# Retention stage of a routed two-layer kernel: row-half scores, decays moved to values and output, diagonal state, routing in groups of blocks

## The reference

```python
# 1 retention, per batch b (2), head h (8), 768 steps, head_dim 64
gamma = 1.0 - 2.0 ** (-5.0 - arange(8))
state = gamma * state + outer(k[t], v[t])
y[t]  = (1 / sqrt(64)) * q[t] @ state
# 2 one expert of eight per token (D 512, F 1024), in token order
fresh = argmax(logits[s])
e     = fresh if s == 0 or local_gate[s] < 0.5 else previous e
out[s] = softmax(logits[s])[e] * relu(x[s] @ w1[e]) @ w2[e]
# 3 four attention experts, top two mixed
```

## Time and profile before

| | us |
|---|---|
| median of three runs | 480.01 |
| lowest and highest run | 478.17, 480.32 |
| span of the profiled execution | 478.0 |
| busy PE, DVE, ACT, POOL | 430.0, 298.3, 211.8, 115.2 |
| the longest chain: PE, DVE, issue, DMA | 74%, 11%, 7%, 4% |

### The profile page before, as it was taken

The page is one execution under the profiler, slowest core; times in us unless marked ns, Lnnn a source line. Parts: engine busy times, 40 slices in busy tenths (PEclk is TensorE's granted clock), DMA queues, the critical chain, the costliest instruction groups (busy, mean ns, idle before and its releaser), DMA issues.

```text
span 478.0 us, 9620 instructions
## 1 busy us (share of the span) xinstructions
PE 430.0 (90%) x3060; PEld 382.2 (80%) x3061; DVE 298.3 (62%) x677; ACT 211.8 (44%) x413; POOL 115.2 (24%) x126
## 2 busy tenths in 40 slices
PE   3899999934999999999999999579979899979887
PEld 2888888824989898989898999379957689967675
DVE  2599999974656565656565654254788841687860
ACT  1123322253346464646464646134555643455653
POOL 1546556320110000000000000170049600014340
PEclk9999999965999999999999999969989999998999
DMA  7987566227777767677776791162400011220003
GB/s 245 300 272 213 180 217 240 106 101 280 236 257 257 263 219 263 224 258 234 256 249 206 240 346 50 49 194 78 121 0 2 2 62 73 66 66 0 0 0 132
DMA packets 32723, 78.37 MB, mean 164 GB/s; under 512 B 4032, under 2 KB 4160, under 8 KB 32704
## 3 DMA queue, kind: packets, MB, share of 16 engines
q1 hardware_dynamic: 25888, 58.21, 37.6%
q0 software_dynamic: 4512, 15.73, 9.7%
q10 hardware_dynamic: 2304, 4.20, 2.3%
HBM read 57.67 MB, written 17.30 MB: 157 GB/s over the span
## 4 chain that ended last, share of the span: by engine, by line
PE 74%; DVE 11%; issue 7%; DMA 4%; ACT 2%; POOL 1%; SPq 1%; DVEq 0%; ACTq 0%; POOLq 0%
PE bank L1188 7%; PE bank L1189 7%; PE bank L1190 7%; PE bank L1205 6%; PE bank L1203 6%; PE bank L1204 6%; PE bank L1303 4%; PE bank L1288 4%; PE bank L1273 2%; PE bank L1082 2%; PE bank L1168 2%; PE bank L1249 2%; PE bank L1247 2%; PE bank L1248 2%; PE bank L1274 2%
## 5 line engine op out<-in xcount | busy, mean ns | idle before, releaser
L1188 PE MATMUL bank<-xh,w1h 128*128 128x256 f32 x256 | 73.5, 287 | 0.9 <-DVE xl L901 0.9
L1189 PE MATMUL bank<-xl,w1h 128*128 128x256 f32 x256 | 73.3, 286 | 0.0
L1190 PE MATMUL bank<-xh,w1l 128*128 128x256 f32 x256 | 73.2, 286 | 0.0
L895 DVE TENSOR_TENSOR w2l<-raw,w2h 128x1024 fp32r<-128x1024 f32 x32 | 37.2, 1222 | 43.0 <-ACT w2h L581 43.0
L518 POOL TENSOR_SCALAR att<-att,stat,mixw 128x128 f32<-128x128 f32 (+5 forms) x48 | 34.1, 718 | 95.0 <-DVE stat L1037 95.0
L581 ACT ACTIVATE w2h<-raw 128x1024 fp32r<-128x1024 f32 x32 | 31.5, 1049 | 47.8 <-PE bank L1205 45.6
L1188 PEld LDWEIGHTS bank<-xh,w1h 128*128 128x128 f32 x256 | 50.0, 195 | 1.3 <-DVE xl L901 1.0
L1203 PE MATMUL bank<-w2h,hh 128*128 128x512 f32 x128 | 50.6, 395 | 0.0
L1189 PEld LDWEIGHTS bank<-xl,w1h 128*128 128x128 f32 x256 | 50.1, 196 | 0.3
L1190 PEld LDWEIGHTS bank<-xh,w1l 128*128 128x128 f32 x256 | 50.0, 195 | 0.0
L1205 PE MATMUL bank<-w2h,hl 128*128 128x512 f32 x128 | 49.9, 390 | 0.0
(11 more groups left out here) (155 smaller groups left out, 975.5 us busy)
## 6 DMA issues: line engine op xcount, KB each, us to landing
raw<-in_w SPq DMA_DIRECT2D x64, 512.0 KB, 6.5
xr<-tokens_by_expert POOLq DMA_DIRECT2D x8, 512.0 KB, 4.1
outputs_by_expert<-ysb ACTq DMA_DIRECT2D x16, 256.0 KB, 5.7
tokens_by_expert<-zero POOLq DMA_DIRECT2D x7, 512.0 KB, 6.2
q_in<-in_qT SPq DMA_DIRECT2D x12, 256.0 KB, 2.8
kz_in<-in_kT SPq DMA_DIRECT2D x24, 128.0 KB, 4.1
k_in<-in_kR SPq DMA_DIRECT2D x12, 256.0 KB, 3.9
v_in<-in_vR SPq DMA_DIRECT2D x12, 256.0 KB, 4.1
```

The costliest lines, as they stand in the source:

```text
L895: dve.tensor_tensor(part(low), raw[:, q, :], part(high).bitcast(F32), ALU.subtract).then_inc(w_lo, 1)
L1188: pe.matmul(to, w1h[:, dc, at], xh[:, dc, :], start=(dc == 0), stop=False)
L1189: pe.matmul(to, w1h[:, dc, at], xl[:, dc, :], start=False, stop=False)
L1190: last = pe.matmul(to, w1l[:, dc, at], xh[:, dc, :], start=False, stop=(dc == DC - 1))
```

## The change

- Scores: the keys are loaded without zeros (`kt_in`), and each head's product has 64 rows, in partitions 0 to 63 or 64 to 127. The heads of a pair go to banks 0 and 1. DVE multiplies all eight heads by one causal mask, in one instruction of 1024 columns.
- Decays: gamma^-s is put on the values by ACT (`v_dec`, eight activations of 64 columns), gamma^t and the scale on the output by DVE, in place of ACT's copy to `xT`. POOL's two multiplications are gone.
- State: 64 x 64 for each head, 256 columns instead of 512. Keys times values and state times queries are eight products of 64 columns or 64 x 64 each instead of four full ones. No state is formed for the last block of a batch, and none read for the first.
- Routing in groups of blocks (0-2, 3-5, 6-8, 9-10, 11). A group's fresh choice is made one block after its last, its scans two blocks after, its places three blocks after. The scans run over up to 384 tokens. The probabilities are computed for all blocks at once, after the first tile is split.
- `xT` and `state` are rings of two, `xrow` is a ring of four.
- POOL writes zeros to the first 256 rows of the token list at the start, and the first tile is loaded when the scatters have landed; the first expert's pad, at row 256 at the earliest, follows. Five zero writes of 512 KB to the outputs, two of SP and three of POOL before, are all on SP's queue behind the first weights.
- The decay constants are 0.35 MB instead of 1.3 MB.

```diff
-        pe.matmul(bank[:, h // 4, ...], kz_in[:, s, par, hp * P:(hp + 1) * P], q_in[:, s, ...])
+        own = half_rows(par)
+        last = pe.matmul(bank[:, par, at], kt_in[own, s, at], q_in[own, s, at], start=True, stop=True)
...
+            def state_out(i):            # 8 products, 64 rows x 64 columns, 128 wide
+                pe.wait_ge(state_ready, states_before(i))
+                        pe.matmul(bank[own, 3, hp * P:(hp + 1) * P], state[own, i % 2, hp, :],
+                                  q_in[own, i % RING, hp * P:(hp + 1) * P], ...)
...
+            for i in range(NB):          # TensorE
+                block_scores(i)
+                if i >= 1:
+                    rows_and_gates(i - 1)          # waits xT_ready i, xrow_ready i-1
+                if i - 2 in closing:
+                    turn_fresh(closing[i - 2])
+                if i - 3 in closing:
+                    turn_places(closing[i - 3])
+                chunk_out(i)                       # state_out(i), then probs x v_dec
+                if i % C < C - 1:
+                    block_kv(i)
+            last_g = len(GROUPS) - 1
+            rows_and_gates(NB - 1)
+            turn_fresh(last_g - 1)
+            turn_places(last_g - 1)
+            turn_fresh(last_g)
+            turn_places(last_g)
...
+            for i in range(NB):          # VectorE
+                mask_scores(i)
+                if i >= 1:
+                    sum_gates(i - 1)
+                block_x(i)
+                if i % C < C - 1:
+                    block_state(i)
+                if i - 1 in closing:
+                    fresh_choice(closing[i - 1])
+                if i - 2 in closing:
+                    count_places(closing[i - 2])
+                if i - 3 in closing:
+                    read_places(closing[i - 3])
...
+            def token_rows(j):           # ScalarE
+                act.wait_ge(gates_ready, j + 1)
+                if j >= XRING:
+                    act.wait_ge(scattered[j % XRING], 16 * (j // XRING))
+                act.activation(xrow[:, j % XRING, :]...).then_inc(xrow_ready, 1)
+            for i in range(1, NB + 1):
+                token_rows(i - 1)
+                if i - 2 in closing:
+                    kept(closing[i - 2])
+                if i + 1 < NB:
+                    decay_values(i + 1)
...
+            for g, (a, z) in enumerate(GROUPS):    # GpSimd
+                pool.wait_ge(pos_ready, g + 1)
+                for j in range(a, z):
+                    pool.wait_ge(xrow_ready, j + 1)
+                    pool.indirect_dma_start(xs, ... posi[:, j:j + 1] ..., xrow[:, j % XRING, :], None)
...
+            for s in range(XRING):                 # SyncE
+                sp.wait_ge(scattered[s], 16 * NB // XRING)
+            sp.dma_start(xr[:, :, :], rows(xs, 0, TILE)...).then_inc(first_tile_in, 16)
             sp.wait_ge(pads_ready, 1)
             sp.dma_start(rows(xs, r, TILE)..., zero[:, :]).then_inc(first_padded, 16)
-            sp.wait_ge(first_padded, 16)
-            sp.dma_start(xr[:, :, :], rows(xs, 0, TILE)...).then_inc(first_tile_in, 16)
```

More of the change, by code:

```diff
@@ L150, in build_kernel @@
[L150 to L160, removed]
+        state = sb("state", [P, 2, HP, HD])
@@ L382, in load_w1 @@
+            for i in range(2, NB):
+                load_turned(i)
+                load_plain(i)
             def load_w1(e, q):
@@ L529, in _, with decay_values @@
         def _(act):
+            def decay_values(i):
+                s, to = i % RING, i % 2
+                act.wait_ge(chunk_in[s], 32 * (i // RING) + 32)
+                if i >= 2:
+                    act.wait_ge(y_done, i - 1)
+                    act.wait_ge(kv_done, states_before(i - 1))
+                for h in range(H):
+                    at = slice(h * HD, (h + 1) * HD)
+                    last = act.activation(v_dec[:, to, at], v_in[:, s, at], ACT.Copy, scale=lead[:, L_KD + h:L_KD + h + 1])
+                last.then_inc(v_ready, 1)
@@ L564, in _ @@
-            with act.Fori(1, NB // RING) as k:
-                for s in range(RING):
-                    i = RING * k + s
-                    token_rows(i - 1, (s - 1) % RING, k - 1 if s == 0 else k)
-                    exps(i - 2, (s - 2) % RING)
-                    route(i - 2, (s - 2) % RING)
-                    retention(i, s)
-            token_rows(NB - 1, RING - 1, NB // RING - 1)
-            exps(NB - 2, RING - 2)
-            route(NB - 2, RING - 2)
-            exps(NB - 1, RING - 1)
@@ new lines, in chunk_out @@
+            def chunk_out(i):
+                pe.wait_ge(xT_ready, i)
+                if i % C:
+                    state_out(i)
+                pe.wait_ge(probs_ready, i + 1)
+                pe.wait_ge(v_ready, i + 1)
+                for hp in range(HP):
+                    for par in range(2):
+                        h = 2 * hp + par
+                        last = pe.matmul(bank[half_rows(par), 3, hp * P:(hp + 1) * P],
+                                         v_dec[:, i % 2, h * HD:(h + 1) * HD], probs[:, par * HP + hp, :],
+                                         start=(i % C == 0 and hp == 0), stop=True, skip_group_check=True)
+                last.then_inc(y_done, 1)
@@ new lines, in block_kv @@
+            def block_kv(i):
+                s = i % RING
+                pe.wait_ge(chunk_in[s], 32 * (i // RING) + 32)
+                pe.wait_ge(state_ready, states_before(i))
+                for hp in range(HP):
+                    for par in range(2):
+                        at = slice((2 * hp + par) * HD, (2 * hp + par + 1) * HD)
+                        last = pe.matmul(bank[half_rows(par), 2, hp * HD:(hp + 1) * HD], k_in[:, s, at],
+                                         v_dec[:, i % 2, at], start=True, stop=True)
+                last.then_inc(kv_done, 1)
@@ L1175, in _ @@
             pe.wait_ge(delta_ready, 1)
-            pe.matmul(bank[:, 7, 0:E], ones[0:1, :], over[0:1, 0:E], start=True, stop=True).then_inc(ey_done, 1)
+            pe.matmul(bank[:, 7, 0:E], ones[0:1, 0:P], over[0:1, 0:E], start=True, stop=True).then_inc(ey_done, 1)
             with pe.Fori(0, E) as e:
```

556 lines of the change are left out of this document (252 added, 304 removed).

## The result

The changed kernel takes 486.38 us (median of 4 runs, 484.02 to 488.18), the kernel before 480.16 on the same chip. The ratio is 1.0131, its 95% interval 1.0090 to 1.0171: slower, by about 6 us. The profiled execution took 484.02 us with a span of 482.4, against the span of 478.0 before. Device times of its runs lie 1.5 to 1.6 us over their spans.

A forecast was written before the change was run, and what follows sets the result against it. Either PE or DVE was taken to set the pace from 41 to 84 us. Start -7.0, middle +6.2 and tail +6.0 gave +5.2, span 478.0 to 483.2, plus 2.0 to the median: 485.2 us, range 474 to 494.

The forecast's parts named there:

- The ring wait: Middle: PE's rows of blocks 5 and 8 wait until scatters free `xrow` slots; stalls of 3.4 and 3.5 us.
- The crowding at block 8: Middle, block 8: first weights and five zero writes in flight lengthen the stall by 1.0 us.
- Start: Up to the end of block 0's output: ends at 11.7 instead of 18.68 us, a gain of 7.0.
- Products: PE's products and turns from block 0's to block 11's output: 64.1 us, with scores at 1.5 a block.
- The middle: End of block 0's output to end of block 11's: 76.9 us before clock losses, 83.0 with them, a loss of 6.2.
- stalls for places: Middle: PE's turn_places waits for DVE's counting, 1.55 us three times, 4.7 in all.
- half clock: Middle: slowed clock costs 2.2 us behind each of two stalls and 1.7 from the start, 6.1 us.
- Tail: Block 11's output to the experts' first product: 26.8 us against 20.8, a loss of 6.0.
- Rival 1: Scores and stage clock: halves overlap whole, scores take 1.02 us and the clock holds; 475 us, chance 0.27.
- Rival 3: State products: a pair's heads don't overlap, 1.8 instead of 1.0 us ten times; 493 us, chance within a shared 0.10.
- Rival 4: Start: scores wait for something else and the 7.0 us gain shrinks; +3 us, chance within a shared 0.10.

The follow-up runs named there:

- the ring of six: The changed kernel with six slots for `xrow` instead of four: 461.85 us, ratio 0.9629 to the kernel before.
- the groups of two: The changed kernel with routing in six groups of two blocks, `xrow` still four slots: 470.54 us; with weights and zero writes also held back, 466.95 us.
- the weights held: The changed kernel with the first expert's weights and the zero writes issued only after the scatters of blocks 1 and 5 landed: 483.09 us.
- the run with both changed: The ring of six, with ACT no longer waiting for plain keys before scaling the first values and its table loaded earlier: 462.66 us.
- busy work in the stalls: The changed kernel with unused identity products on PE before rows_and_gates of blocks 5, 8 and 11: 483.83 us.
- after: The changed kernel itself, with the whole change against the kernel before: 486.38 us, ratio 1.0131.

## Why the prediction was right

The sign, the place and the size were right: 485.2 predicted, 486.38 measured. That it came so close is in part luck. The start gained 2.6 us less than predicted, the middle lost 2.1 less and the tail 1.4 less. Inside the middle the products came out 10.0 us shorter and the ring stalls 6.8 us longer than predicted. The mechanism, saved products that come back as waits for a slot, is what the runs show.

- **The ring wait decides**: shown, by the ring of six (20.7 us of waits for ACT's copy to none, 24.5 us of time) and by the groups of two. Its size at block 5 was 5.4 against the 3.4 predicted: from block 5's output DVE's steps ahead of the scatter took 1.7 (1.0 predicted), the scatter 4.0 (3.2) and the copy 0.75 (0.66), and PE's scores ahead of the wait were shorter (1.1, not 1.5), which lengthens a stall that ends at a fixed moment. At block 8 it was 9.5 against 3.5 and the 1.0 for crowding.
- **The crowding at block 8** was the worst-sized term: 1.0 predicted, 4.6 less in the stall with the weights held (3.3 in the time). I charged it as a small share of 16 us of traffic; the scatter started just behind 2 MB of weights and took 8.4 us from start to release.
- **Start**: 4.4 gained, not 7.0. The scores took 2.08 us, 2.85 predicted, but I took the scaled values as ready. I had not read what ACT's wait asks for, nor looked for the table load behind it; the run with both changed had the output at 11.97. (The prediction's steps add up to 11.6 and not 11.7.)
- **Products.** Scores 1.09: row halves overlap nearly whole (the bound was 1.02), 4.5 us in eleven blocks. Keys times values 0.56, not 1.0: 4.4 us. Values times scores 0.92, 1.4 us. The turns took 0.75 each, 0.6 less in all; rows and state were 0.9 over. In all 54.1, or 10.0 us less than my 64.1.
- **The middle** then closes: 54.1 of products, 4.35 of stalls for places (1.37, 1.49, 1.49; predicted 4.7), 14.9 of ring stalls (8.1 predicted), and 7.6 left for half clock and small gaps (6.1 predicted): 80.9. Rows at half the clock make 5.8 of this: 0.7 behind block 0, 1.4 where the clock fell at 39.4, 1.6 behind each of the two ring stalls, and 0.5 at 94.1. So a stall cost 1.6 in slow rows and not 2.2, the start 0.7 and not 1.7, and two falls of the clock lay where I had none. Against the ring of six the middle is longer by 80.9 - 62.9 = 18.0, the two stalls and 3.1 beside their length. Of that, busy work in the stalls won back 2.5 at most: ACT's queue is late there too.
- **Tail** 25.4 against 26.8, along the steps predicted: rows 5.84 after block 11's output (5.95), two counts, the last scatter 15.7 after it (16.8). The 1.4 us less come from the first count and its turn, over at T + 12.0 and not at 13.1.
- **Rival 1** (halves overlap whole, the clock holds) was half right: they overlap, the clock didn't hold, and every product shortened ahead of a ring stall came back in the stall. The 3.4 us that it gives to the scores don't follow from its own numbers: 0.48 in eleven blocks is 5.3, and half of it 2.6.
- **Rival 3** is refuted. State times queries of a pair's two heads, in two opposite quarters of the array, both write bank 3. Sixteen records take 1.03 us, 64 ns each, as line 1105 did, and in the trace's single records the products of a pair start 7 ns apart, the next pair 110 ns later. The Trainium skill, TensorEngine Tiling (Array Packing), Gotcha 1: PSUM Pressure, says that different row tiles cannot access one bank at once; the measurement differs, for products of 64 x 64. Nor do loads of 128 columns into different row halves follow one another: sixteen scores' loads take 0.97 us, where the prediction's estimate from the Trainium skill, TensorE: Matmul & The Clock Gate, LDWEIGHTS, was 1.7.
- **Rival 4** came true in small, for a reason that I had not named: what ACT waits for, and its table, cost some 2.4 us of the start.

What stays open: why the clock falls where it does (at 55.7 and 76.2 in the run that had started 2.4 us earlier, at 84.5 in the ring of six); and how much of a scatter's landing, 2.7 to 8.5 us, is chance (block 0's took 4.0 and 5.5 us to its release in two kernels with the same program up to there).

## What to carry to other kernels

When work is grouped, a buffer is released later by the length of the group and by all that follows it: recount every ring against the new latest release, in blocks. Here four slots for groups of three made three stalls of 20.7 us together, about what the products of the middle save (PE is busy with them for some 75 us before and 54 after), and two more slots were worth 5%. Holding back a crowding transfer can move the crowding to the next small one, as with groups of two. Read each semaphore wait of a moved operation for what it asks beyond its operands, and look up which transfers are issued just ahead of a small one that something waits for.

## What the runs showed of the hardware

- Two products of 64 rows in different row halves overlap, weight loads of 128 columns too: sixteen records in 1.09 us (68 ns each), against 1.88 us with 128 rows. The two of a pair start 6 to 7 ns apart, the next pair 110 ns later, and with 128 rows each record starts 112 ns behind the one before. Keys times values, 64 columns wide on either side, takes 35 ns a record.
- POOL's multiplication slowed DVE's 8x128 step from 0.34 to 1.92 us: with POOL's cut to one column it is 0.34 in every block. POOL's own scatter issue then has a median of 0.99 us, and 0.96 in after, where it was 1.65.
- An indirect scatter of 256 KB landed in 2.7 us with little beside it and in 8.5 behind 2 MB of weights; with these held back the same one took 3.8 us from its start to the release.
- Eight activations of 64 columns take 2.02 us, 250 ns each, and a first activation on ACT another 1.28 for its table, behind the wait that stands before it.
